# Clustered attention before two feed-forward blocks: the mean of V for empty rows by constant columns beside the probabilities, pairs of PSUM banks used in turn, and new orders on all engines

## What is computed

```python
# q, k, v: (2, 8, 768, 64); centroids: (8, 16, 64); float32
q_assign = np.argmax(np.einsum('bhsd,hcd->bhsc', q_n, c_n), axis=-1)
k_assign = np.argmax(np.einsum('bhsd,hcd->bhsc', k_n, c_n), axis=-1)
mask = q_assign[:, :, :, None] == k_assign[:, :, None, :]
scores = scale * np.matmul(q, k.transpose(0, 1, 3, 2))
scores = np.where(mask, scores, -1000000000.0)
scores = scores - np.max(scores, axis=-1, keepdims=True)
attn = np.exp(scores)
attn = attn / (np.sum(attn, axis=-1, keepdims=True) + 1e-09)
return np.matmul(attn, v).astype(np.float32)
```

## Time and profile before

| | us |
|---|---|
| median of three runs | 778.05 |
| the profiled execution | 778.41 |
| its span, first to last instruction | 776.5 |
| TensorE busy in it | 754.8 |
| VectorE, ScalarE, GpSimd busy in it | 442.7, 386.8, 352.9 |
| start of the trace to turn_maxima of step 1 | 55.08 |
| twelve steps from there (turn_maxima of step 1 to that of step 13) | 178.59 |
| tail, to the start of rational_products | to 274.53 |
| the rest, the two feed-forward blocks | to 776.5 |

### The profile page before, as it was taken

The page is one execution under the profiler, slowest core; times in us unless marked ns, Lnnn a source line. Parts: engine busy times, 40 slices in busy tenths (PEclk is TensorE's granted clock), DMA queues, the critical chain, the costliest instruction groups (busy, mean ns, idle before and its releaser), DMA issues.

```text
span 776.5 us, 10055 instructions
## 1 busy us (share of the span) xinstructions
PE 754.8 (97%) x3601; PEld 571.2 (74%) x3601; DVE 442.7 (57%) x731; ACT 386.8 (50%) x652; POOL 352.9 (45%) x285
## 2 busy tenths in 40 slices
PE   4799999999999999999999999999999999999998
PEld 2565665655656678888888888878888888888886
DVE  6788788888875476777767687674332101210210
ACT  4356665666665778887666677762211011010101
POOL 5177887887887746752222223443322201210220
PEclk9699999999999999999999999999999999999999
DMA  8534444444431442000000032601000010001001
GB/s 180 153 89 102 113 111 107 103 103 115 99 95 35 130 130 74 1 2 0 1 1 1 0 109 95 230 22 61 28 1 1 0 42 14 1 16 38 0 0 54
DMA packets 54481, 47.70 MB, mean 61 GB/s; under 512 B 29274, under 2 KB 45690, under 8 KB 54436
## 3 DMA queue, kind: packets, MB, share of 16 engines
q1 hardware_dynamic: 54436, 47.12, 21.8%
HBM read 28.35 MB, written 3.15 MB: 41 GB/s over the span
## 4 chain that ended last, share of the span: by engine, by line
PE 94%; ACT 1%; DVE 1%; DMA 1%; issue 1%; POOL 1%; SPq 0%; DVEq 0%; ACTq 0%; POOLq 0%
PE psum L826 91%; PE psum L831 2%; DMA RAWQK<-in_k 1%; PE psum L583 1%; ACT OPS L1080 0%; PE psum L897 0%; POOL PSUMS L1520 0%; DVE MROW L1334 0%; ACT P L1111 0%; POOL G L512 0%; SPq L735 0%; DVE psum L1294 0%; DVE psum L1334 0%; ACT OPS L1073 0%; ACT OPS L1068 0%
## 5 line engine op out<-in xcount | busy, mean ns | idle before, releaser
L826 PE MATMUL psum<-OPS 128*128 128x384 f32 x576 | 132.9, 363 | 9.8 <-issue 5.1
L826 PEld LDWEIGHTS psum<-OPS 128*128 128x128 f32 x576 | 99.4, 195 | 45.6 <-issue 20.6
L826 PE MATMUL psum<-XT,W 128*128 (+1 forms) x576 | 131.0, 389 | 0.0
L512 POOL TENSOR_TENSOR G<-TT,G 128x512 fp32r<-128x512 f32 x48 | 62.5, 1302 | 149.8 <-ACT G L402 149.8
L826 PEld LDWEIGHTS psum<-XT,W 128*128 128x128 f32 x576 | 108.1, 188 | 22.5
L1520 POOL TENSOR_TENSOR PSUMS<-PSUMS,P 128x768 f32<-128x768 f32 x64 | 117.3, 1833 | 5.6 <-ACT P L1111 1.0
L1111 ACT ACTIVATE P<-psum 128x768 f32<-128x768 f32 x96 | 77.9, 811 | 67.6 <-PE psum L826 66.7
L1334 DVE TENSOR_REDUCE psum<-psum 128x1 f32<-128x768 f32 x90 | 86.8, 965 | 38.4 <-PE psum L826 36.3
L697 DVE TENSOR_TENSOR ABF<-AS,psum 128x512 f32<-128x512 f32 x24 | 16.5, 688 | 146.8 <-ACT AS L671 146.8
L721 POOL TENSOR_TENSOR W<-ABF,W 128x512 fp32r<-128x512 f32 x24 | 31.0, 1290 | 147.2 <-DVE W L701 147.2
L826 PE MATMUL psum<-G,WSPLIT 128*128 128x512 f32 x360 | 86.5, 390 | 1.1 <-POOL G L512 1.1
(11 more groups left out here) (117 smaller groups left out, 1074.8 us busy)
## 6 DMA issues: line engine op xcount, KB each, us to landing
OPS<-OPS SPq DMA_DIRECT2D x32, 192.0 KB, 3.0
W3R<-in_moe_w SPq DMA_DIRECT2D x8, 512.0 KB, 3.7
W12RAW<-in_moe_w SPq DMA_DIRECT2D x8, 512.0 KB, 4.2
RAWQK<-in_q SPq DMA_DIRECT2D x16, 192.0 KB, 3.2
RAWQK<-in_k SPq DMA_DIRECT2D x16, 192.0 KB, 3.4
V<-in_v SPq DMA_DIRECT2D x16, 192.0 KB, 2.5
XT<-XH SPq DMA_DIRECT2D x32, 96.0 KB, 2.4
XT<-XL SPq DMA_DIRECT2D x32, 96.0 KB, 2.2
```

Of the source, the lines that this page charges most:

```text
L512: nc.gpsimd.tensor_tensor(G[:, n % 2, 1, :], TT[:, n % 4, :], G[:, n % 2, 0, :].bitcast(F32), ALU.subtract).then_inc(g_lo, 1)
L826: return nc.tensor.matmul(o, stationary, moving, start=start, stop=stop, skip_group_check=True)
```

## The change

1. P32 gets two more columns beside each half of 384, set once to 2^-50 / 768; probs_v multiplies 386 columns instead of 384, now one tile (four records) at a time, so that column 384 of VO becomes V's sum times that constant. take_out copies this column to VMEAN and adds it to all of VO as the bias of an activation. sum_v, empty_values, v_over_tiles, round_v_sums, split_v_sums and the flag columns go; place_maxima and the fifth copy of place_masks handle one row instead of three. The constant in the sum (EMPTY_SUM) is 2^-50 instead of 1e-9.
2. PAIR_A and PAIR_B (the former TP and ST) are shared by scores, sides and similarities: in steps 1 to 13 scores 0, 1, 2 and 5 go to A, scores 3 and 4 to B, sides and similarities of u >= 4 to B, and the turned maxima of units 2 to 14 to A. The waits follow: scores(u, 3) waits for rest_of_q and rest_of_k of u + 3, scores(u, 4) for turn_similarities(u + 3), scores(u, 5) for copy_maxima(u + 1).
3. All orders are new. On TensorE probs_v comes in groups with sums or similarities; the clusters of u + 3 are finished within step u (before: in step u + 1), and place_masks runs for u + 3; on SP load_v comes last and load_qk first in a step; in the start-up sides(3) comes ahead of score_max(0, 0), and the early weights are loaded after copy_rows(2) and load_qk(4).

The diff, cut to its core (the start-up, the tail, buffers and semaphores follow the same lines):

```diff
-            P32 = ph("P32", [P, 4, S], F32)
+            P32 = ph("P32", [P, 4, 2, HALF + 2], F32)
...
+        PAIR_A, PAIR_B = TP[:, :, 0:HALF], ST
         def sides_banks(u):
-            return ST if u in (1, 2) else TP[:, :, 0:HALF]
+            return PAIR_A if u in (0, 3) else PAIR_B
         def sims_bank(u):
-            return VO if u in (1, 2) else TP[:, 0, 0:HALF]
+            return VO if u in (1, 2) else PAIR_A[:, 0] if u in (0, 3) else PAIR_B[:, 0]
+        def score_banks(u, n):
+            return PAIR_A if 1 <= u <= UNITS - 3 and n in (0, 1, 2, 5) else PAIR_B
+        def turn_bank(u):
...
             load_qk(0)
             load_qk(1)
-            load_v(0)
             load_qk(2)
+            sp.dma_start(COEF[:, 0:4], a.rearrange("(o n) -> o n", o=1).partition_broadcast(P)).then_inc(ld_coef, 16)
+            sp.dma_start(COEF[:, 4:6], b.rearrange("(o n) -> o n", o=1).partition_broadcast(P)).then_inc(ld_coef, 16)
             copy_rows(0)
             copy_rows(1)
             load_qk(3)
+            load_v(0)
+            copy_rows(2)
+            load_qk(4)
             for f in range(EARLY_W):
                 load_weights(sp, f, ld_early)
-            copy_rows(2)
-            sp.dma_start(COEF[:, 0:4], a.rearrange("(o n) -> o n", o=1).partition_broadcast(P)).then_inc(ld_coef, 16)
-            sp.dma_start(COEF[:, 4:6], b.rearrange("(o n) -> o n", o=1).partition_broadcast(P)).then_inc(ld_coef, 16)
             place_maxima(0)
+            place_masks(2)
+            place_maxima(1)
+            load_v(1)
+            copy_rows(3)
+            place_masks(3)
...
             def step(u):
-                load_v(u + 1)
+                if has(u + 4):
+                    load_qk(u + 4)
                 if has(u - 2):
                     place_x(u - 2)
-                if has(u + 2):
-                    place_masks(u + 2)
                 if has(u + 3):
                     copy_rows(u + 3)
                 place_maxima(u + 1)
-                if has(u + 4):
-                    load_qk(u + 4)
-            for u in range(UNITS - 1):
+                if has(u + 3):
+                    place_masks(u + 3)
+                load_v(u + 1)
+            for u in range(1, UNITS - 2):
                 step(u)
...
+                if u >= 4:
+                    pe.wait_ge(exp_done, NT * (u - 3) + 4)
...
+                    if n == 0:
+                        pe.wait_ge(nm_copied if u <= 2 else nm_ready, u)
+                    pe.wait_ge(sm_free, NT * u + n)
...
-                nc.tensor.transpose(SM[:, 0, 0:P], NM.bitcast(F32), IDENT).then_inc(sm_ready, 1)
+                if 2 <= u <= UNITS - 2:
+                    pe.wait_ge(exp_done, NT * (u - 1) + 3)
+                nc.tensor.transpose(turn_bank(u), NM.bitcast(F32), IDENT).then_inc(nm_turned, 1)
...
+                elif n == 0:
+                    if u == 1:
+                        pe.wait_ge(sims_read, 4)
+                    else:
+                        pe.wait_ge(exp_done, NT * u)
+                elif n in (1, 2):
                     pe.wait_ge(exp_done, NT * u + n)
+                elif n == 3:
+                    if has(u + 3):
+                        pe.wait_ge(q_lo, u + 4)
+                        pe.wait_ge(k_lo, u + 4)
+                    else:
+                        pe.wait_ge(exp_done, NT * u - 1)
+                elif n == 4:
+                    if has(u + 3):
+                        pe.wait_ge(sims_read, u + 4)
+                    else:
+                        pe.wait_ge(exp_done, NT * u + 4)
+                else:
+                    pe.wait_ge(nm_copied, u + 2)
                 for which_k, which_q in ((BK, BQ), (AK, AQ)):
                     for x in range(2):
-                        last = mm(ST[:, x], ops(u, which_k)[:, n * P:(n + 1) * P],
+                        last = mm(score_banks(u, n)[:, x], ops(u, which_k)[:, n * P:(n + 1) * P],
...
+            def probs_v(u, n):
+                if n == 0:
+                    pe.wait_ge(ld_v[u % 2], 16 * (u // 2) + 16)
+                    if u == 0:
+                        pe.wait_ge(sims_read, 3)
+                        pe.wait_ge(consts_set, 1)
+                    else:
+                        pe.wait_ge(v_out, u)
+                pe.wait_ge(exp_done, NT * u + n + 1)
+                for x in range(2):
+                    last = mm(VO_MEAN[x * D:(x + 1) * D], V[:, u % 2, n, :], P32[:, (2 * u + n) % 4, x, :], n == 0, n == NT - 1)
                 last.then_inc(pv_done, 1)
...
             def step(u):
                 scores(u, 0)
-                probs_v(u - 1, 2)
+                if has(u + 3):
+                    sides(u + 3)
                 score_max(u + 1, 3)
                 scores(u, 1)
-                if has(u + 3):
-                    sides(u + 3)
-                empty_values(u)
+                sums(u - 1)
+                probs_v(u - 1, 5)
                 score_max(u + 1, 4)
                 scores(u, 2)
-                sums(u - 1)
+                scores(u, 3)
                 score_max(u + 1, 5)
-                scores(u, 3)
                 probs_v(u, 0)
+                probs_v(u, 1)
+                if has(u + 3):
+                    similarities(u + 3)
+                score_max(u + 2, 0)
                 turn_maxima(u + 1)
                 scores(u, 4)
-                score_max(u + 2, 0)
-                if has(u + 3):
-                    similarities(u + 3)
                 scores(u, 5)
                 score_max(u + 2, 1)
-                probs_v(u, 1)
-                sum_v(u + 1)
+                for n in (2, 3, 4):
+                    probs_v(u, n)
                 score_max(u + 2, 2)
...
                 if has(u - 1):
                     act.wait_ge(nm_rows, 16 * u)
-                nc.scalar.copy(NMT[0:3 * NT, :], SM[0:3 * NT, 0, 0:P]).then_inc(sm_free, 1)
+                nc.scalar.copy(NMT[0:NT, :], turn_bank(u)[0:NT]).then_inc(nm_copied, 1)
...
                 if n >= 4:
-                    act.wait_ge(pv_done, BATCHES * u + 1)
+                    act.wait_ge(pv_done, NT * u + n - 3)
                     act.wait_ge(p_added, (NT - 1) * u + 1)
                 elif has(u - 1):
-                    act.wait_ge(pv_done, BATCHES * (u - 1) + 2 + n // 2)
+                    act.wait_ge(pv_done, NT * (u - 1) + n + 3)
                     act.wait_ge(p_added, (NT - 1) * (u - 1) + 2 + n)
-                nc.scalar.activation(P32[:, (2 * u + n) % 4, :].rearrange("p (h n) -> p h n", h=2), ST, ACT.Exp,
+                nc.scalar.activation(P32[:, (2 * u + n) % 4, :, 0:HALF], score_banks(u, n), ACT.Exp,
...
-                nc.scalar.copy(VOUT, VO).then_inc(v_out, 1)
+                nc.scalar.copy(VMEAN, VO_MEAN[:, HALF:HALF + 1]).then_inc(v_mean, 1)
+                act.wait_ge(v_mean, u + 1)
+                nc.scalar.activation(VOUT, VO, ACT.Identity, bias=VMEAN).then_inc(v_out, 1)
...
             def step(u):
                 exponent(u, 0)
-                round_v_sums(u)
+                if has(u + 3):
+                    round_k(u + 3)
+                    round_q(u + 3)
+                exponent(u, 1)
+                reciprocal_sums(u - 1)
                 take_out(u - 1)
-                if has(u + 2):
-                    scale_masks(u + 2)
-                exponent(u, 1)
-                if has(u + 3):
-                    round_q(u + 3)
-                    round_k(u + 3)
                 exponent(u, 2)
-                reciprocal_sums(u - 1)
                 exponent(u, 3)
+                round_x(u - 1)
+                if u <= 2 * EARLY_W:
+                    split_early_hi(act, u)
                 copy_maxima(u + 1)
                 exponent(u, 4)
                 exponent(u, 5)
-                if u <= 2 * EARLY_W:
-                    split_early_hi(act, u)
-                round_x(u - 1)
+                if has(u + 3):
+                    scale_masks(u + 3)
...
+            nc.vector.memset(P32[:, :, :, HALF:HALF + 2], EMPTY_SUM / S).then_inc(consts_set, 1)
...
+                    dve.wait_ge(nm_turned, u)
+                nc.vector.tensor_scalar(NM[:, 0:NT], rows, -1.0, CAP, ALU.mult, ALU.min).then_inc(nm_ready, 1)
...
             def step(u):
-                if has(u + 2):
-                    write_one_hot(u + 2)
-                    turn_one_hot(u + 2)
-                split_v_sums(u)
                 row_max(u + 1, 3)
+                if has(u + 3):
+                    rest_of_k(u + 3)
+                    rest_of_q(u + 3)
                 row_max(u + 1, 4)
-                if has(u + 3):
-                    rest_of_q(u + 3)
+                divide_first(u - 1)
                 row_max(u + 1, 5)
+                divide_last(u - 1)
                 negate_maxima(u + 1)
                 if has(u + 3):
-                    rest_of_k(u + 3)
-                divide_first(u - 1)
+                    turn_similarities(u + 3)
                 row_max(u + 2, 0)
-                divide_last(u - 1)
```

(40 more changed lines are left out.)

294 lines of the change are left out of this document (114 added, 180 removed).

## The result

The changed kernel takes 783.49 us, median of four runs (782.55 to 785.69); the kernel before, on the same chip, 777.87 (776.86 to 778.56). The ratio is 1.0077, 95% interval 1.0053 to 1.0102: slower by 5.6 us, where I had forecast 770.8, faster by 7. The profiled execution is the slowest of the four, 785.69 with a span of 783.8.

The account below looks back on a forecast made before the run. A ring of waits through SP's queue was to pace steps at 14.55 us instead of 14.88: 4.0 gained, plus 1.0 step 13, 1.0 tail, 1.3 start-up, 7.3 off 778.41, so 771.1; median 770.8, range 760 to 778.5.

Parts of the forecast that it names:

- the ring: Attention steps: wait loop from turn_one_hot through SP's queue, x's landing, round_x, copy_maxima and scores(u, 5), pacing steps at 14.53 us.
- three short waits: TensorE's step: waits at scores 1, similarities and scores 4, some 0.5 us on top of 13.42, giving 13.9.
- the sum of 771.1: Whole kernel: profiled execution of 778.41 us less 7.3 gained in the steps, step 13, tail and start-up.
- landing of x: Each step: last x copy lands 2.2 us after its issue, up to 2 us later if queued behind loads.
- the low end of the masks: SP's queue: four mask copies take 2.51 us to issue, not up to 3.54, given a pause ahead of them.
- the case called Slower: Steps: x copies queue behind V, q and k, round_x 1 to 1.5 us later, steps of 15.5, 782 us; chance 0.11.
- the 15.15 from which I had it decide: Step length, 14.88 + 3.3 / 12, from which the kernel was expected to be slower than before.
- the 3.3 that I had forecast as gained elsewhere: Outside the twelve steps: 1.0 us from step 13, 1.0 from the tail and 1.3 from the start-up.
- The start-up: Before the steps: a gain of 1.3 us, range -1.5 to 2.5, from removed matmuls, against later weights, sides(3) and clock.
- if the start lost more than 2 us: Start-up: a loss above 2 us was named as a sign that the prediction is wrong.
- Step 13 and tail: End of attention: 1.0 us gained in step 13 (0 to 1.2) and 1.0 in the tail (0 to 1.4).
- The weighed rule: TensorE: changing tiling mode drains it, so one saved switch would partly remain; own work 13.5 to 13.7 us, not 13.42.

Follow-up runs that it names:

- the run of 765.47: Changed kernel with round_x and weight split behind exponent 5, early weights ahead of copy_rows(2), sides(3) behind score_max(0, 0), load_qk(4) behind place_maxima(0): 765.47 us, ratio 0.9833.
- the last run: Kernel of the run of 765.47 with, in SP's queue, place_x ahead of load_qk and load_v ahead of place_masks as well: 766.0 us, ratio 0.9832.
- the run of 767.73: Changed kernel with round_x and the early weight split moved behind exponent 5 on ScalarE: 767.73 us, ratio 0.9871.
- the two start-up edits: Kernel of the run of 767.73 with early weight loads ahead of copy_rows(2) and load_qk(4), and sides(3) behind score_max(0, 0): 767.32 us, ratio 0.9864.
- the run of 849.6: Changed kernel with place_x(u - 1) moved ahead of place_masks(u + 3) in SP's queue: 849.62 us, ratio 1.0929.
- the run of 780.98: Changed kernel with only the weight split moved from ahead of copy_maxima to behind exponent 5 on ScalarE: 780.98 us, ratio 1.0053.

## Why the prediction was wrong

**The frame held.** The prediction named the ring, its links and that it paces, and the page shows each link. TensorE's own step with three short waits was put at 13.9; it is 13.94, though the matmuls show only 0.06 of idle in it, so that the 0.5 for the waits is not shown. The mask waits of before are gone. V waits once, for 0.2. ScalarE's added column copy is 0.14 and covered. The profiled execution, itself 2.2 above the median, came out 14.6 us above the sum of 771.1: 9.8 in the steps, 4.5 in the start-up, 0.3 elsewhere.

**The step that failed: the ring's length, taken at its low end.** For the step shown above, from the end of turn_one_hot at 78.47 to the next at 94.18, 15.71 instead of 14.53:

| term | predicted | measured |
|---|---|---|
| turn_one_hot to the first mask | 0.60 | 0.55 |
| SP's queue to the last x issue | 6.93 | 7.45 |
| landing of x | 2.2 | 3.15 |
| round_x, split, copy_maxima | 1.52 | 1.32 |
| scores(u, 5) to turn_one_hot | 3.28 | 3.24 |
| together | 14.53 | 15.71 |

The landing is four fifths of the error. I had taken 2.2 from a page row of before, where one load of V, not three loads, stood ahead of the copies, and had written beside it "up to 2 us later if they queue behind them". The row was right for its neighbours and wrong for the new ones. In the queue the masks took 2.83 for 2.51 and V 0.57 for 0.33, while the row took 0.57 for 0.81; my reason for the low end of the masks, a pause ahead of them, held in part only: they took 2.83 here and 2.53 in the next step. This is the mechanism of the case called Slower, in the right place and at its price: steps of 15.5 there, and here nine turns of 15.64, 15.5 without the clock's part (below). Step 1 and the last steps don't wait for the ring, so the twelve steps are 15.37 in the mean, still over the 15.15 from which I had it decide. They lost 5.8 us against the 3.3 that I had forecast as gained elsewhere: slower by 2.5, and by 1.1 if all of the clock's part is taken off. The start-up, below, added the rest. I gave the case 0.11, because its only support was an upper bound that I had set myself. The range of 14 to 16 for the ring was fair, and twelve steps turn each of its tenths into 1.2 us: the total should have reached past 783.

**A term that I had at nothing: the clock inside the steps.** Two steps of the profiled execution took 17.28 and 17.16 where others with the same wait took 15.7. TensorE's timeline there:

```profile
106.63 1.71 PE L833 MATMUL psum<-OPS 128*128 128x384 f32 x6 [1.47 <-ACT NMT L1124]
108.27 3.38 PE L833 MATMUL psum<-P,V 128*64 128x386 f32 x12
```

And by stretch, the stall, and what follows it:

```profile
105.10:106.60 1.50, 0.07 (x1) 0.00 (x0) 1.28 (x4) 1.21 (x4) 0.00 (x0) 1.00 0.15 35
...
108.00:110.00 2.00, 2.00 (x8) 0.77 (x8) 1.59 (x3) 0.55 (x1) 1.86 (x2) 0.50 0.01 1
```

Twelve P·V take 3.38, and 2.17 in other steps: the granted clock between 108 and 110 is 0.50, 1.2 of 2.4 GHz. In the kernel before the twelve steps were at 1.00. Yet it would be wrong to charge 1.5 us for each of the two steps. The P·V don't lie in the ring, and the turns of the ring, from copy_maxima to copy_maxima, hardly feel the first fall:

```profile
106.33 0.25 ACT L1124 CAST NMT<-psum 6x128 fp32r<-6x128 f32 x1
...
121.75 0.25 ACT L1124 CAST NMT<-psum 6x128 fp32r<-6x128 f32 x1
...
137.48 0.25 ACT L1124 CAST NMT<-psum 6x128 fp32r<-6x128 f32 x1
```

These two turns take 15.42 and 15.73, and what TensorE lost in the step of 17.28 it had back in the next, of 13.94, in which it waited for nothing. What the falls cost is what they add inside the ring, from copy_maxima to the start of scale_masks: 3.93, 3.81 and 4.29 at 106.33, 121.75 and 137.48, where it is 3.56 at 90.64. That is 0.37, 0.25 and 0.73, at most 1.4 of the 9.8. Without it the nine turns are (140.79 - 1.35) / 9 = 15.5.

**The start-up: +3.2 instead of -1.3.** I had charged nothing of "0 to 1.5" for place_maxima(0) behind the weights. It landed 4.9 after its issue, and the first scores began at 33.11; in the run of 765.47, at 30.70. The start-up runs show that what was issued ahead of it delays it, the weights in one case, q and k of unit 4 in the other; with the weights issued by 23.0 and q, k behind it, the 3.2 us are gone in the one execution of that kernel that was profiled, and 1.3 of them are left in that of the last run, with the same start-up. The data of sides(3) were late as well (3.40 idle ahead of it, score_max(0, 0) at 19.76 for 17.43). I had called that hidden by VectorE, and it was not quite: turn_maxima(0) comes at 26.69 in the run of 767.73, and at 25.58 with the two start-up edits. Those 1.1 us were then lost again to the landing. A part was the clock: of the 3.5 between the changed kernel and the run of 765.47 at the turn of step 1, 2.4 stand at the first scores and 1.1 behind them, where groups still ran at the low clock (the granted clock is 0.50 from 33 to 39 in the changed kernel, and 0.95 from 34 to 36 in that run). I had given this 0 to 1 in the prediction. My range for the start-up, up to 1.5 slower, left out that all could come together, and "if the start lost more than 2 us" was the sign of being wrong that I had named.

**Step 13 and tail: -2.1 for -2.0.** The sum is right; how it splits between the two was not read.

**The weighed rule.** Sums and P·V now share one entry: 81.74 to 83.19 is 1.45, two times 0.645 and 0.15. P·V with similarities don't:

```profile
85.49 1.52 PE L833 MATMUL psum<-P,V 128*64 128x386 f32 x8
86.94 0.85 PE L833 MATMUL psum<-OPS,CT 128*32 128x384 f32 x8
87.72 0.62 PE L833 MATMUL psum<-OPS 128*128 128x384 f32 x2
```

Similarities take 0.78 from start to start. In the run with the columns alone they stand behind full-width scores, and take the same:

```profile
83.95 0.85 PE L819 MATMUL psum<-OPS,CT 128*32 128x384 f32 x8
84.73 1.32 PE L819 MATMUL psum<-OPS 128*128 128x384 f32 x6
```

So P·V ahead of them saves none of their entry. The Trainium skill (TensorEngine Tiling (Array Packing), Key Properties) says that a change of tiling mode drains TensorE; going from 64 columns to 32 is such a change, and the trace agrees as far as it goes: 0.78 either way. TensorE's own work is then, as an estimate, 13.42 and one entry of 0.15, 13.57, in the 13.5 to 13.7 that I had given for that case; the step measured is 13.94. The two columns more cost about their share: a group of eight P·V goes 1.45 from start to start, and 1.44 before.

## What to carry to other kernels

A buffer with one owner, waited for by an in-order engine, ties every queue between its last reader and that wait into one ring; when steps are reordered, add up the ring by its links and look at who stands behind the wait, then cut it there: a second buffer, the waiting instruction moved last, or the release moved ahead of the loads in its queue each gave some 16 us here. A long step of one engine is no loss by itself while a ring paces: measure from one passage of the ring to the next. Take a small DMA's landing from a row with the same transfers ahead of it, and put large loads behind what an engine waits for. And before a DMA group is moved in a queue, look up when its data are ready on every engine that makes them.

## What the runs showed that I had not expected

- The landing of a 96 KB copy depends on what was issued just ahead: in the medians of the runs 2.1 to 2.2 behind other small copies, 2.9 to 3.3 behind V, q and k of 192 KB each, 2.2 again when these were cut in halves. At the start-up a copy of six rows landed after 4.9 with the weights just ahead, after 5.8 with q and k just ahead, and after 3.6 and 4.3 with both moved away; in the kernel before the first scores began 2.2 after its issue. What makes up that last difference stays open.
- After stalls of 1.4 to 1.5 us TensorE's clock fell to its lower level in two of the steps and not in two others with stalls of 1.46 and 1.49, nor after one of 2.12. Behind the 5 us stalls of the run of 849.6 it was 0.72 in the mean over 115 to 121 and over 136 to 142 us. The stall's length alone doesn't decide it here. What does, and how often it happens in executions that weren't profiled, stays open. The run of 780.98 had no fall, with its longest such stall 1.71. In every kernel without these stalls the twelve steps were at 1.00.
